# First attention chunk's low halves moved from GpSimd to VectorE, semaphores, a bank and a tile count moved at the two expert layers

## The chip, the cores and the metric

The kernel runs on one core of a Trainium2 chip. The metric is device time in microseconds, lower is better. The four engines that compute (TensorE, VectorE, ScalarE, GpSimd) and SyncE, which issues most transfers, each work through an own queue in program order and meet at semaphores: an instruction waits until a semaphore has reached a value, and raises one when it ends. Chunk, block and tile are used below as the kernel's own units.

## The reference

Three stages, each on 9984 rows of 256 values:

```python
# B=4, S=2496, D=256, z of width 64
attn = maximum(z @ z.T / S, 0) ** 2          # for each of the 4 batches
x    = u * (attn @ v)

# first expert layer: 8 experts, hidden width 1024
do   = x @ w_skip > 0                         # rows that are computed; others pass unchanged
e    = argmax(x @ w_gate);  g = softmax(...)[e]
x    = x + g * (relu(x @ w1[e]) @ w2[e])      # only where do

# second expert layer: the gate has a bias by the row's modality (0 or 1)
e    = argmax(x @ w_gate2 + bias[modality]);  g = softmax(...)[e]
out  = g * (relu(x @ w1b[e]) @ w2b[e])
```

## The kernel before, in words

**Precision.** All large products are made from float32 operands that are split in two parts: a high part, which is a rounding copy (`VH`, `ZH`, `AH`), and a low part, which is the operand minus the high part (`VL`, `ZL`, `AL`). A product is three matmuls: high by high, high by low, low by high. So each operand needs a copy on some engine and a subtraction on some engine.

**Attention.** There are 20 chunks, 5 for each batch; a chunk is 512 columns of the output (448 for a batch's last). The other side is taken in 20 blocks of 128, two at a time, so that a chunk has 10 pairs `p`. For a pair TensorE makes the scores (`scores`, line 1567, six matmuls into `pS`), ScalarE applies ReLU (`relus`, line 742) and square (`squares`, line 751) to each block, VectorE splits each block in `AH` (line 1183) and `AL` (line 1185, in `split`), and TensorE sums `V` times `A` (`sums`, `half_sums`, line 1578; twelve matmuls a block). TensorE runs three pairs ahead with its scores (`AHEAD`). Scores of a pair wait for the ReLUs of the pair before. ScalarE's square of a block waits until VectorE has split the block four before it.

**Where V comes from.** `V` of a batch lies in 20 blocks, cast and subtracted two at a time (index `n`, 0 to 9). SyncE loads batch 0 in five pieces: blocks 0 and 1, blocks 2 and 3 (semaphores `v_first_loaded`), blocks 4 to 9 (`v_loaded`), blocks 10 to 15 (`v_mid_loaded`, issued once `vl_ready` has reached 3, because the raw buffer is reused), and 16 to 19 (issued at `vl_ready` 5). In chunk 0 VectorE makes the high parts: `v_high(0)` before chunk 0's loop, the others after the splits of a pair, as the table `V_AT` says (line 1188). GpSimd makes all ten low parts (`v_low`, line 579), each as soon as its high part is there. TensorE's sums of pair `p` wait for `vl_ready` p + 1. For batches 1 to 3 ScalarE makes the high parts and VectorE the low parts, in both versions. The five parts of `Z` are cast by ScalarE (`z_high`) and subtracted by VectorE (`z_low`) in both.

**First expert layer.** Rows that go to one expert lie together in `token_rows`, and are taken in tiles of 256. The first tile ("lead") is made by `lead_layer1` and `lead_layer2`, written out by hand among the last routing steps; hidden units come in four banks. `lead_layer2(n, bank)` waits for the `n`-th raise of `h_split`. How many tiles each expert has is counted on VectorE (`finish_groups(0)`), which raises `cum_ready`; every engine then reads the counts with `value_load` (line 323 in `end_of`) and loops. On TensorE the order is `lead_layer2(2, 1)`, wait for `cum_ready`, read the first count, `lead_layer2(3, 3)`, loop (layer 1 at line 1834, layer 2 at line 1851).

**Second expert layer.** Tiles of 512, in `second_phase` of each engine. TensorE makes tile 0 with `layer1` (line 1886) into the banks `hring_lead` = pT, pS1, pS0 by turns, and `layer2` (lines 1894 and 1896). Eight blocks `f` of hidden units; `layer1(t, ..., f)` waits for `q.h_split`, which VectorE raises by `NF` = 8 at the head of its own `second_phase` (line 1465), and by one with each `h_low`. Before the second `layer1`, TensorE waits for the last output of the first layer (`PH[0].y_out`; it frees pS1), and behind it come three small matmuls (`prefix_x2`, line 1805) that wait for the one-hot of the last first-layer tile, which VectorE makes in `pick_expert` (lines 1383 to 1392) after it has read a count (line 1492). `place_tile`, `finish_groups(1)` and the low halves follow on VectorE. Counts of the second layer go to SyncE, which pads the end of an expert's rows and then loads tile 1 (`load_x`, line 429). TensorE turns the rows of tile 1 with `transpose_half` (line 1877), half by half, into pT, ScalarE (`take_half`) and VectorE (`low_half`) split them. Before the first half it waits for `h_split` NF + 7, with which VectorE has read pT's last block.

Of the kernel before, what the change touches and what calls it, by code (L numbers as in the profile page):

```python
# [5 lines left out]
F32 = mybir.dt.float32  # L6
# [4 lines left out]
ALU = mybir.AluOpType  # L11
# [5 lines left out]
B, S, D, DQ = 4, 2496, 256, 64  # L17
# [6 lines left out]
KP = KT // 2  # L24
# [5 lines left out]
VU = KT // 2  # L30
# [4 lines left out]
FIRST = 4  # L35
# [3 lines left out]
VHALF = KT // 2  # L39
VMID = VHALF + 6  # L40
# [7 lines left out]
NF = F // P  # L48
# [19 lines left out]
def bass_attention_two_moe(nc, u, v, z, w_skip, w_gate, w1, w2, modality, w_gate2, bias2, w2t, out):  # L68
    xs = nc.dram_tensor("token_rows", (GR * CAP + SPARE, ROW), F32, kind="Internal").ap()

    with ExitStack() as ctx:
# [430 lines left out]
        def _(pool):  # L502
            g_ = nc.gpsimd

            def wait(semaphore, value):

                pool.wait_ge(semaphore, value)
                pool.sem_inc(pool_passed, 1)
# [66 lines left out]

            def v_low(n):
                to, at = 2 * n * D, 2 * (n % (VU // 2)) * D
                wait(vh_ready, n + 1)
                g_.tensor_tensor(VL[:, to:to + 2 * D], vraw[:, at:at + 2 * D], VH[:, to:to + 2 * D].bitcast(F32), ALU.subtract).then_inc(vl_ready, 1)

            def row_meta(idx):
# [14 lines left out]
            pool.sem_inc(x_ready, 2)  # L596
            for n in range(VU):
                v_low(n)
            for g in range(CHUNKS):
# [71 lines left out]
        def _(act):  # L671
# [87 lines left out]
            for g in range(CHUNKS):  # L759
                b, c = divmod(g, QC)  # L760
                n = TAIL if c == QC - 1 else QW
                for p in range(KP):
# [8 lines left out]
                    if g == 0 and p in (1, 2, 4):  # L771
                        z_high(0, 2 + p // 2)
                    if p in MIDDLE and b < B - 1:
                        m = MIDDLE.index(p)
# [130 lines left out]
            def second_phase():  # L905
# [35 lines left out]
                for f in range(NF):  # L941
                    h_high(0, f, hring_lead)
                    if 3 <= f < 3 + WP:
                        split_high(E + 1, 1, f - 3)
                take_half(1, 0, 0, pT[:, :])
                take_half(1, 0, 1, pT[:, :])
                keep_marks(1, 0)
# [47 lines left out]
        def _(dve):  # L995
# [171 lines left out]
            def v_high(n):  # L1167
                w, at = slice(2 * n * D, 2 * (n + 1) * D), 2 * (n % (VU // 2)) * D
                if 2 * n < FIRST:
                    dve.wait_ge(v_first_loaded[n], 16)  # L1170
                elif VHALF <= 2 * n < VMID:
                    dve.wait_ge(v_mid_loaded, 16)
                else:
                    dve.wait_ge(v_loaded, 16 if 2 * n < VHALF else 64)
                v_.tensor_copy(VH[:, w], vraw[:, at:at + 2 * D]).then_inc(vh_ready, 1)
# [11 lines left out]

            V_AT = {0: (1,), 1: (2, 3), 2: (4,), 4: (5,), 5: (6, 7), 6: (8,), 7: (9,)}
            final_done = [0]
# [53 lines left out]

            z_low(0, 0)
            v_high(0)
            z_low(0, 1)
            for g in range(CHUNKS):
                n = TAIL if g % QC == QC - 1 else QW
                for p in range(KP):
                    split(g, p, n)  # L1250
                    if g == 0:
                        if p in (1, 2, 4):
                            z_low(0, 2 + p // 2)
                        for m in V_AT.get(p, ()):
                            v_high(m)
                    else:
# [47 lines left out]
            dve.sem_inc(PH[0].h_split, 4)  # L1304
            dve.sem_inc(PH[0].y_out, 1)
            dve.wait_ge(u_loaded, 16 * CHUNKS)
# [155 lines left out]
            def second_phase():  # L1462

                q = PH[1]
                dve.sem_inc(q.h_split, NF)
                dve.sem_inc(q.y_out, 1)

# [33 lines left out]
                for f in range(3, NF):  # L1501
                    h_low(0, f, hring_lead)
                low_half(1, 0, 0, pT[:, :])
                low_half(1, 0, 1, pT[:, :])
                dve.wait_ge(marks_loaded, 16)
# [38 lines left out]
        def _(pe):  # L1544
# [246 lines left out]
            for ph in range(1):  # L1791
# [4 lines left out]
                gate_columns(1)  # L1796
                lead_layer2(2, 1)
                pe.wait_ge(cum_ready, ph + 1)
                first_end = end_of(pe, 0, 0)
                lead_layer2(3, 3)  # L1800

# [65 lines left out]
            def second_phase():  # L1867
# [66 lines left out]
                layer2(0, 0, 4)  # L1934
                pe.wait_ge(q.h_split, NF + 7)
                transpose_half(1, 0, pT)
                layer2_last(0, 0, lambda: transpose_half(1, 1, pT))
                pe.wait_ge(cum_ready, 2)
# [62 lines left out]
```

## Time and profile before

| what | us |
|---|---|
| timed runs, median of 3 | 1475.42 (1475.3 to 1476.66) |
| profiled execution | 1478.75 |
| its span | 1477.20 |
| TensorE busy | 1454.6 (98%) |
| VectorE busy | 980.9 (66%) |
| ScalarE busy | 778.2 (53%) |
| GpSimd busy | 278.9 (19%) |
| granted TensorE clock, share of full speed | 0.998 |

The span is the time from the first to the last instruction of the profiled execution; 1.55 us lie around it. The profiled execution is 3.3 us over the median of the timed ones. In the rows PE is TensorE's matmuls and PEld its weight loads, DVE is VectorE, ACT ScalarE, POOL GpSimd, SP SyncE; a name with q behind it is an engine's queue of register, branch and semaphore instructions. A bracket [0.28 <-ACT R L742] says that the engine stood idle for 0.28 us before the row and what ended that. "issue" is a wait that no semaphore in the profile explains. The ends of matmuls are modelled.

### The profile page before, as it was taken

The numbers are of one execution on the slowest core, as the hardware profiler recorded it, in microseconds if no ns is written. First come the engines' busy times: TensorE is split into PE (matmuls) and PEld (weight loads), VectorE is DVE, ScalarE is ACT, GpSimd is POOL, SyncE is SP. The second block draws the span as 40 slices with busy tenths as digits, with TensorE's granted clock in tenths as the row PEclk, the third lists the DMA queues.
The fourth block names the chain that finished last, engine by engine and source line by source line (L and its number), as shares of the span: only waits on it lengthen the run. The fifth ranks groups of instructions, "written<-read, shape, count | busy, mean of one in ns | idle before, by whom it ended". The sixth has DMA issues, their size and how long they took to land.

```text
span 1477.2 us, 34369 instructions
## 1 busy us (share of the span) xinstructions
PE 1454.6 (98%) x11832; PEld 1312.6 (89%) x11832; DVE 980.9 (66%) x2487; ACT 778.2 (53%) x1540; POOL 278.9 (19%) x309
## 2 busy tenths in 40 slices
PE   9999999999999999999999999999999999999997
PEld 7889998999998898889899999997888888888885
DVE  7988888888788888888676666674333333333332
ACT  6677767677667677666444444444333333333332
POOL 4011111111111111111332222225121121211212
PEclk9999999999999999999999999999999999999999
DMA  5311030201311111031464344323111121111110
GB/s 122 101 52 45 30 101 29 66 31 43 101 63 39 38 50 67 31 102 58 131 211 131 129 142 133 107 97 124 47 43 47 40 73 43 43 47 40 58 44 26
DMA packets 59066, 108.01 MB, mean 73 GB/s; under 512 B 18615, under 2 KB 33474, under 8 KB 58940
## 3 DMA queue, kind: packets, MB, share of 16 engines
q1 hardware_dynamic: 40396, 47.46, 11.5%
q0 software_dynamic: 18544, 58.96, 11.4%
q8 instruction: 69, 1.13, 0.3%
q14 instruction: 57, 0.47, 0.1%
HBM read 75.61 MB, written 32.31 MB: 73 GB/s over the span
## 4 chain that ended last, share of the span: by engine, by line
PE 95%; issue 2%; DVE 1%; ACT 0%; DMA 0%; SPq 0%; POOLq 0%; DVEq 0%; POOL 0%; ACTq 0%
PE pO L1578 33%; PE pS L1886 11%; PE pO L1894 10%; PE pS L1567 9%; PE pS L1851 9%; PE pO L1834 9%; PE pO L1896 5%; PE pM L1886 4%; PE pT L1877 1%; PE pO L1587 1%; PE pM L1650 1%; DVE AH L1183 1%; PE pT L1769 1%; PE pO L1751 0%; PE pS L1738 0%
## 5 line engine op out<-in xcount | busy, mean ns | idle before, releaser
L1578 PE MATMUL pO<-AH,VH 64*128 64x512 f32 (+1 forms) x1520 | 323.8, 383 | 0.8 <-DVE AL L1185 0.5
L1578 PE MATMUL pO<-AH,VL 64*128 64x512 f32 (+1 forms) x1520 | 322.9, 382 | 1.7 <-issue 1.7
L1578 PE MATMUL pO<-AL,VH 64*128 64x512 f32 (+1 forms) x1520 | 323.1, 382 | 0.0
L742 ACT ACTIVATE R<-pS 128x512 f32<-128x512 f32 (+1 forms) x400 | 213.7, 589 | 168.3 <-PE pS L1567 165.6
L1185 DVE TENSOR_TENSOR AL<-A,AH 128x512 fp32r<-128x512 f32 (+1 forms) x400 | 278.9, 697 | 13.7
L751 ACT ACTIVATE A<-R 128x512 f32<-128x512 f32 (+1 forms) x400 | 228.2, 626 | 9.0 <-DVE AL L1185 9.0
L1894 PE MATMUL pO<-VL,AH 128*128 128x512 f32 x640 | 232.2, 400 | 0.0
L1183 DVE CAST AH<-A 128x512 fp32r<-128x512 f32 (+1 forms) x400 | 170.5, 426 | 45.7 <-ACT A L751 45.2
L1578 PEld LDWEIGHTS pO<-AH,VH 64*128 64x128 f32 x1520 | 172.2, 184 | 15.8 <-issue 1.5
L1578 PEld LDWEIGHTS pO<-AH,VL 64*128 64x128 f32 x1520 | 172.4, 184 | 15.2 <-issue 2.9
L1578 PEld LDWEIGHTS pO<-AL,VH 64*128 64x128 f32 x1520 | 172.4, 184 | 12.5
L1477 DVE SCALAR_TENSOR_TENSOR AL<-pS,AH 128x512 fp32r<-128x512 f32 x119 | 82.2, 691 | 150.9 <-ACT AH L924 150.9
L1896 PE MATMUL pO<-VL,AL 128*128 128x256 f32 x640 | 179.1, 280 | 0.0
L1886 PE MATMUL pS<-ZH,VH 128*128 (+1 forms) x476 | 160.6, 391 | 0.0
L924 ACT ACTIVATE AH<-pS 128x512 fp32r<-128x512 f32 x119 | 71.2, 599 | 163.4 <-PE pS L1886 134.0
L631 POOL DMA_INDIRECT out_dram<-xrow,tok_at x80 | 78.1, 977 | 366.7 <-DVE xrow L1487 354.3
L1894 PEld LDWEIGHTS pO<-VL,AH 128*128 128x128 f32 x640 | 120.2, 188 | 26.4
L1896 PEld LDWEIGHTS pO<-VL,AL 128*128 128x128 f32 x640 | 120.4, 188 | 2.4
L1834 PE MATMUL pO<-ZH,VH 128*128 x704 | 117.3, 284 | 0.1
L1851 PE MATMUL pS<-VL,AH 128*128 128x264 f32 x704 | 116.0, 287 | 0.0
L1886 PEld LDWEIGHTS pS<-ZH,VH 128*128 128x128 f32 x476 | 89.4, 188 | 20.3
L1834 PEld LDWEIGHTS pO<-ZH,VH 128*128 128x128 f32 x704 | 98.5, 191 | 1.4 <-issue 1.4
(276 smaller groups left out, 2387.4 us busy)
## 6 DMA issues: line engine op xcount, KB each, us to landing
raw<-in_w_dram POOLq DMA_DIRECT2D x22, 1024.0 KB
A<-token_rows SPq DMA_DIRECT2D x20, 536.0 KB
uT<-in_u_dram SPq DMA_DIRECT2D x16, 512.0 KB, 3.7
xin<-token_rows SPq DMA_DIRECT2D x23, 268.0 KB
raw<-in_v_dram SPq DMA_DIRECT2D x8, 768.0 KB
A<-in_w2t_dram POOLq DMA_DIRECT2D x8, 512.0 KB
raw<-in_z_dram SPq DMA_DIRECT2D x8, 368.0 KB, 5.0
token_rows<-pad_row SPq DMA_DIRECT2D x8, 268.0 KB
```

Of the source, the lines that this page charges most:

```text
L742: s_.activation(R[k % 2][:, 0:n], pS[k % 2][:, 0:n], ACT.Relu, scale=1.0 / S).then_inc(relu_done, 1)
L751: s_.activation(A[k % NA][:, 0:n], R[k % 2][:, 0:n], ACT.Square).then_inc(square_done, 1)
L1183: v_.tensor_copy(AH[k % NBUF][:, 0:n], A[k % NA][:, 0:n]).then_inc(ah_ready, 1)
L1185: v_.tensor_tensor(AL[k % NBUF][:, 0:n], A[k % NA][:, 0:n], AH[k % NBUF][:, 0:n].bitcast(F32), ALU.subtract).then_inc(al_ready, 1)
L1477: v_.scalar_tensor_tensor(out=AL[f][:, :], in0=ring[f % RING][:, :], scalar=0.0, in1=AH[f][:, :].bitcast(F32), op0=ALU.max, op1=ALU.subtra ...
L1567: last = t_.matmul(pS[r][:, 0:n], w[rows, (2 * p + r) * P:(2 * p + r + 1) * P], x[rows, zc:zc + n], start=(m == 0), stop=(m == 2))
L1578: last = t_.matmul(pO[:, (KD * r + d) * QW:(KD * r + d) * QW + n], vv[rows, vo + k * D + d * P:vo + k * D + (d + 1) * P], a[k % NBUF][rows ...
L1834: last = t_.matmul(pO[:, bank * 512 + fi * TT:bank * 512 + (fi + 1) * TT], w[h][:, kd, f * P:(f + 1) * P], x[:, ds(par, 1), kd, :].rearran ...
L1851: last = t_.matmul(pS[s][:, 0:width], a[p][:, fi * TT + s * P:fi * TT + (s + 1) * P], w[h][:, f, 0:width], start=(f == 0 and n == 0), stop ...
L1886: last = t_.matmul(ring[f % RING][:, :], w[h][:, kd, f * P:(f + 1) * P], x[:, ds(par, 1), kd, :].rearrange("p o t -> p (o t)"), start=(n = ...
L1894: t_.matmul(pO[:, s * QW:(s + 1) * QW].rearrange("p (m d) -> p m d", m=2), AH[f][:, rows], w2hl[h][:, :, f, 0:D], start=(f == 0), stop=(f ...
L1896: return t_.matmul(pO[:, s * QW:s * QW + D], AL[f][:, rows], w2h[h][:, f, 0:D], start=False, stop=(f == NF - 1), skip_group_check=True)
```

## The change

1. Attention, chunk 0: GpSimd's ten `v_low` are gone. VectorE makes them in its own order, `v_low(0, 0)` before its loop and `v_low(0, p + 1)` after the splits of pair p. VectorE keeps `v_high(0)` and `v_high(1)`; the high parts 2 to 9 are made by ScalarE, `v_high(0, p + 1)` after the squares of pair p, for p = 1 to 8.
2. VectorE raises `PH[1].h_split` by 8 and `PH[1].y_out` by 1 before the first expert layer, no longer at the head of `second_phase`.
3. Tile 1 of the second layer is turned into pM instead of pT. TensorE's wait before it is for `PH[0].base` of the last first-layer tile (pM's last reader) instead of `h_split` NF + 7.
4. TensorE makes `lead_layer2(3, 3)` before it waits for `cum_ready` and reads the first count.

```diff
...
@@ GpSimd @@
-            def v_low(n):
-                to, at = 2 * n * D, 2 * (n % (VU // 2)) * D
-                wait(vh_ready, n + 1)
-                g_.tensor_tensor(VL[:, to:to + 2 * D], vraw[:, at:at + 2 * D], VH[:, to:to + 2 * D].bitcast(F32), ALU.subtract).then_inc(vl_ready, 1)
...
-            for n in range(VU):
-                v_low(n)
@@ ScalarE, chunk loop @@
                     if g == 0 and p in (1, 2, 4):
                         z_high(0, 2 + p // 2)
+                    if g == 0 and 1 <= p < KP - 1:
+                        if p == 1:
+                            act.wait_ge(vh_ready, 2)
+                        v_high(0, p + 1)
@@ ScalarE, second layer @@
-                take_half(1, 0, 0, pT[:, :])
-                take_half(1, 0, 1, pT[:, :])
+                take_half(1, 0, 0, pM[:, :])
+                take_half(1, 0, 1, pM[:, :])
@@ VectorE @@
             def v_high(n):
...
-                if 2 * n < FIRST:
-                    dve.wait_ge(v_first_loaded[n], 16)
-                elif VHALF <= 2 * n < VMID:
-                    dve.wait_ge(v_mid_loaded, 16)
-                else:
-                    dve.wait_ge(v_loaded, 16 if 2 * n < VHALF else 64)
+                dve.wait_ge(v_first_loaded[n], 16)
...
-            V_AT = {0: (1,), 1: (2, 3), 2: (4,), 4: (5,), 5: (6, 7), 6: (8,), 7: (9,)}
...
             z_low(0, 0)
             v_high(0)
+            v_low(0, 0)
             z_low(0, 1)
...
-                        for m in V_AT.get(p, ()):
-                            v_high(m)
+                        if p == 0:
+                            v_high(1)
+                        if p < KP - 1:
+                            v_low(0, p + 1)
...
             dve.sem_inc(PH[0].h_split, 4)
-            dve.sem_inc(PH[0].y_out, 1)
+            dve.sem_inc(PH[1].h_split, NF)
+            for q in PH:
+                dve.sem_inc(q.y_out, 1)
...
                 q = PH[1]
-                dve.sem_inc(q.h_split, NF)
-                dve.sem_inc(q.y_out, 1)
...
-                low_half(1, 0, 0, pT[:, :])
-                low_half(1, 0, 1, pT[:, :])
+                low_half(1, 0, 0, pM[:, :])
+                low_half(1, 0, 1, pM[:, :])
@@ TensorE @@
                 lead_layer2(2, 1)
+                lead_layer2(3, 3)
                 pe.wait_ge(cum_ready, ph + 1)
                 first_end = end_of(pe, 0, 0)
-                lead_layer2(3, 3)
...
-                pe.wait_ge(q.h_split, NF + 7)
-                transpose_half(1, 0, pT)
-                layer2_last(0, 0, lambda: transpose_half(1, 1, pT))
+                pe.wait_ge(PH[0].base, total0 + 1)
+                pe.sem_inc(pe_passed, 1)
+                transpose_half(1, 0, pM)
+                layer2_last(0, 0, lambda: transpose_half(1, 1, pM))
```

## Rows read from the trace of the kernel before

**Rows 1.** The page's part 4: shares of the chain that ended last, by engine
```profile
PE 95%; issue 2%; DVE 1%; ACT 0%; DMA 0%; SPq 0%; POOLq 0%; DVEq 0%; POOL 0%; ACTq 0%
```

**Rows 2.** The chain in order of time: start us, us, engine, group
```profile
49.87 3.06 PE pO L1578 x24
...
56.33 0.68 PE pS L1567 x6
...
732.90 4.38 PE pS L1851 x36
```

**Rows 3.** Timeline of TensorE, chunk 0: start us, us, engine, line, operation, count [idle before]
```profile
11.08 0.51 PE L1578 MATMUL pO<-AH,VH 64*128 64x512 f32 x2
...
14.65 0.46 PE L1567 MATMUL pS<-ZH 64*128 64x512 f32 x2
...
17.24 0.50 PE L1567 MATMUL pS<-ZH 64*128 64x512 f32 x2 [0.28 <-ACT R L742]
...
19.41 0.45 PE L1567 MATMUL pS<-ZH 64*128 64x512 f32 x2
```

**Rows 4.** Timeline of VectorE, chunk 0
```profile
15.86 0.76 DVE L1175 CAST VH<-raw 128x512 fp32r<-128x512 f32 x2
...
20.12 0.69 DVE L1185 TENSOR_TENSOR AL<-A,AH 128x512 fp32r<-128x512 f32 x1
```

**Rows 5.** Groups by line and shape, first 60 us: busy us, mean ns, idle
```profile
L1185 DVE TENSOR_TENSOR AL<-A,AH 128x512 fp32r<-128x512 f32 x30 | 27.6, 919 | 1.0
...
L579 POOL TENSOR_TENSOR VL<-raw,VH 128x512 fp32r<-128x512 f32 x10 | 13.3, 1337 | 20.8 <-DVE VH L1175 20.8
```

**Rows 6.** TensorE at the count of the first layer: its queue's load, then its timeline
```profile
L323 PEldq TENSOR_LOAD <-cum x1: 572/572/572, 720.8 to 720.8; - x1
...
721.80 0.33 PE L1738 MATMUL pS<-VL,AH 128*128 128x264 f32 x1
...
724.99 0.39 PE L1834 MATMUL pO<-ZH,VH 128*128 x2
```

**Rows 7.** Timelines of TensorE and VectorE, start of the second layer
```profile
1002.79 0.50 PE L1886 MATMUL pT<-ZH,VH 128*128 128x512 f32 x1 [1.34 <-DVEq L1465]
...
1003.73 0.17 DVE L1383 TENSOR_SCALAR take<-xrow 128x2 f32<-128x2 f32 x1 [0.74 <-DVE xrow L1456]
...
1005.25 0.17 DVE L1392 TENSOR_TENSOR oh<-eq,take 128x16 bf16<-128x16 f32 x1
```

**Rows 8.** Timeline of TensorE and waits of SyncE's queue, before tile 1
```profile
1022.54 0.63 PE L1877 MATMUL pT<-ident,A 128*128 128x128 f32 x4 [1.23 <-issue]
...
SPq L439 <- DVE pad_from L1342: 13.6, 1, 13.6
```

**Rows 9.** Windows: from:to us, length, busy PE, PEld, DVE, ACT, POOL, PEclk, DMA, GB/s
```profile
8.00:9.00 1.00, 0.57 (x10) 0.40 (x8) 0.74 (x1) 1.00 (x3) 0.34 (x1) 1.00 0.93 220
...
13.90:14.00 0.10, 0.10 (x6) 0.06 (x4) 0.10 (x1) 0.10 (x2) 0.00 (x0) 1.00 0.11 31
...
1021.90:1022.00 0.10, 0.00 (x0) 0.00 (x0) 0.00 (x0) 0.00 (x0) 0.10 (x1) 1.00 0.22 86
```

**Rows 10.** Timeline of ScalarE, chunk 0
```profile
14.45 1.15 ACT L751 ACTIVATE A<-R 128x512 f32<-128x512 f32 x2
...
15.49 0.62 ACT L721 CAST ZH<-raw 128x512 fp32r<-128x512 f32 x1
...
16.00 1.10 ACT L742 ACTIVATE R<-pS 128x512 f32<-128x512 f32 x2
...
16.97 1.17 ACT L751 ACTIVATE A<-R 128x512 f32<-128x512 f32 x2
```

**Rows 11.** VectorE's queue at the start of the second layer, lines 1465 and 1492
```profile
L1465 DVEq EVENT_SEMAPHORE  x1: 21/21/21, 1002.7 to 1002.7; - x1
...
L1492 DVEq TENSOR_LOAD <-cum x1: 310/310/310, 1002.9 to 1002.9; - x1
```

**Rows 12.** TensorE's queue, line 323, the second layer's count
```profile
L323 PEldq TENSOR_LOAD <-cum x1: 336/336/336, 1025.5 to 1025.5; - x1
```

## The prediction

> **What bounds the kernel now.** I read the page first, then the chain in order of time, then the timelines of single engines where TensorE stands. The chain that ended last is TensorE for 95% [rows 1]. So only time in which TensorE stands still, or in which its matmuls come further apart than they must, can be won. There are three such places that the change touches.
>
> Place one is the first attention chunk. The chain in order of time runs through VectorE there, and TensorE takes it over only at 49.87 us, with the first sums of chunk 1; from then on a set of six matmuls (scores of two blocks, or half of one block's sums) takes 0.68 us without a break [rows 2]. TensorE's first sums start at 11.08 [rows 3]. Between the two lie 50 such sets: 8 of scores before chunk 1's, 3 of chunk 1's, and 39 of sums (16 blocks of 2, and 7 single ones for the last four blocks). 50 x 0.683 = 34.1 us; they take 38.8, so 4.7 us are lost. Why, a timeline row and a group say: a subtraction on VectorE takes 0.69 us by itself [rows 4], but 0.919 on average over the first 60 us, in which GpSimd makes its ten subtractions of 1.34 us each [rows 5]. 30 x 0.23 = 6.9 us of VectorE's time go there.
>
> Place two is the end of the first expert layer's first tile, at 721 to 725 us: TensorE's sequencer reads the tile count for 0.57 us, and the twelve matmuls behind it take from 721.80 to 724.99, where line 1834 starts [rows 6]. Matmuls of that kind take 0.12 us (4.38 for 36) [rows 2], so 1.46; 1.7 us are lost.
>
> Place three is the start of the second layer: 1.34 us of idle before 1002.79, released by VectorE's semaphore at line 1465 [rows 7], and 1.23 us before the turning of tile 1 at 1022.54 [rows 8].
>
> **Part 1, chunk 0: 0.7 us won.** GpSimd's ten subtractions go. VectorE gets them: 10 x 0.69 = 6.9 us; it gives up 8 casts (two take 0.76, so 3.0) [rows 4] and the 6.9 us of stretching. A pair of blocks then costs it 2 x (0.4 + 0.69) for the splits and 0.69 for the subtraction, 2.9 us, under TensorE's 5 x 0.683 = 3.4. VectorE stops being the bound.
>
> But ScalarE now makes the eight casts, and its queue is in order: the cast of V's third piece stands ahead of the ReLUs of blocks 4 and 5, and must wait for that piece's load. The load is not waited for in the old trace. Its last bytes move at 13.9 to 14.0 us [rows 9]; later, tile 1's load ends at 1022.0 and TensorE, which waited for it, starts at 1022.54 [rows 8, 9], so half a microsecond passes from bytes to semaphore. I take 14.5. The bounds are 14.0 (no delay) and 15.86, where VectorE casts the same piece without having waited [rows 4].
>
> From there, with ScalarE's steps of 0.97 for two ReLUs, 1.04 for two squares, 0.51 for a cast [rows 10], and 0.15 from a ReLU's end to the scores:
> cast at 14.5, ReLUs 4 and 5 from 15.0 to 16.1, next scores at 16.25 (before: 14.65);
> squares 15.97, casts 17.0 and 17.5, ReLUs 18.0 to 19.1, next scores at 19.27 (before: 17.24);
> squares 19.0, cast 20.0, ReLUs 20.5 to 21.6, next scores at 21.8 (before: 19.41) [rows 3].
> TensorE idles for about 1.5, 0.9 and 0.4 us, where it idled 0.28 once. After that ScalarE needs 2.0 + 0.5 + at most 0.5 us in each 3.4 and runs ahead; V's later pieces are asked for no later than now, since the subtraction that frees the raw buffer ends by about 16.3 in these steps, and GpSimd's could not start before the cast at 15.86 and took 1.34. So from 21.8 there are 40 sets left: 21.8 + 0.08 + 40 x 0.683 = 49.2, against 49.87. Won: 0.7, and by the bounds 1.2 or a loss of 0.7. Nothing later absorbs it: up to the end of the first layer TensorE is the chain.
>
> The gaps in that stretch leave TensorE busy for 4.1 of 7 us. A row nearby: from 8 to 9 us it was busy 0.57 of the time and the granted clock was 1.00 [rows 9]. I therefore charge nothing for the clock. The Trainium skill (TensorE: Matmul & The Clock Gate, section HAM oscillation) says that idle gaps between bursts of matmuls can put the array back to the lower of its two rates. By that rule this part would lose; the trace does not agree so far, and the rival below has its price.
>
> **Part 2, the second layer's start: 0.2 us won.** The idle 1.34 us goes, but not the time. The first of the freed steps starts at about 1001.5 and needs 1.5 us; the next waits for the last tile's output, which VectorE ends at 1002.99 (the 0.74 us before the row at 1003.73 count from there), so it starts at 1003.15 and ends at 1004.6. Then comes the prefix matmul, which waits for the one-hot that VectorE ends at 1005.42 [rows 7]. In the old trace it ran at 1005.66 (1002.79 + 1.50 + 6 x 0.228), with nothing to wait for. So the wait moves to the one-hot. What is really won is VectorE's: its two semaphore instructions (0.1 us each, from 1002.7 to the count's load at 1002.9) no longer stand before that load [rows 11], so the one-hot, the counts and all that hangs on them come 0.2 us sooner. Bounds: 0 and 0.4.
>
> **Part 3, the other bank for tile 1: 0.** The stall ends with tile 1's rows, not with a free bank. SyncE waits for VectorE's counts [rows 8], pads, and loads; the last bytes come at 1022.0 [rows 9]. Bank and wait change nothing of that. TensorE's new wait (the first layer's last base) is long met by then, and pM's next writer, the third matmul block of tile 1, already waits for both splits. The 0.2 us above pass through, and no more: had TensorE come earlier it would have stood longer here.
>
> **Part 4, the count read later: 0.5 us won.** The nearest row for "load behind the matmuls, loop next" is the second layer's own count, at 1025.5: 0.34 us, fully hidden by queued matmuls [rows 12]. That speaks for all of the 1.7 us. Against it: the sequencer's load, its twelve pairs of instructions and the loop's entry are one queue whose sum stays the same; only if the stutter comes from the load itself is it saved, and the load is 0.57 of it. An empty queue at the loop's entry could cost that 0.57, with the register work behind it 0.9. I take 0.5, between 1.7 won and 0.9 lost, near the 0.57 of the load's own row [rows 6]. What is late next, the second tile's load, is not near.
>
> **Sum.** 0.7 + 0.2 + 0 + 0.5 = 1.4 us. The profiled execution took 1478.75 us (span 1477.20 and 1.55 around it), so it would take 1477.35. The timed runs, whose median is 1475.42, are 3.3 us below it; the difference carried over gives 1474.0. About 0.2% (3 us) is what a measurement of this kernel can tell from no change.
>
> **Rivals.**
> A, the cover is thinner: the load lands at the upper bound, or ScalarE's chain takes a little more per step, and part 4 costs 0.2. Then +0.7 - 0.2 + 0.2 = +0.7: 1476.1. For it: chunk 0's first 10 us have no slack on ScalarE. Chance 0.18.
> B, all of it comes: the load is early (1.2), part 2 gives 0.3, the stutter was the load's (1.7): 3.2 us, 1472.2. For it: the row at 1025.5. Against it: three independent ends of three ranges. Chance 0.15.
> C, slower: the clock falls in chunk 0 between 14.5 and 22 us. About 5.5 us of matmuls there would take twice as long, +5.5 - 1.4 = +4.1: 1479.5. It decides from the point at which the row of the granted clock goes below 1. Against it: 1.00 in every slice, also at 0.57 busy. Chance 0.06.
> D, the change doesn't do what it says at the second layer's start, since the one-hot takes over the wait: this is my forecast, and the rival that the 1.34 us are won whole (a further 1.1, so 1472.9) has 0.04; the rest is the forecast, 0.57.
>
> **The numbers.** 1474.0 is the likeliest case. Its own range is about 1472.8 to 1475.4. For 8 in 10 I take in A and most of B: 1471.9 to 1476.8. Faster by over 0.2% (under 1472.5) needs nearly all of B: 0.14. Slower needs C or something unseen: 0.06. Within: 0.80.
>
> **What would show it.** In chunk 0 ScalarE idle before its first cast of V (line 733) until about 14.5; TensorE gaps near 16, 19 and 22 and none from there to 60; VectorE's subtractions all at 0.69; chunk 1's first sums near 49.2. At the second layer: no idle before its first matmul, a short one at the second step and about 0.7 before the prefix, which stays near the one-hot's end; the stall before tile 1's turning still over 1 us. At the first layer: line 1834 starting up to 1.7 us sooner after the last block (B) or not (A). Wrong would be a granted clock under 1, a TensorE gap in chunk 0 after 25 us, or a second layer that starts over 0.5 us sooner against VectorE's last tile.

## The result and the profile after

The changed kernel takes 1478.24 us (median of 17 runs, 1476.70 to 1480.58) against 1475.30 (17 runs, 1474.45 to 1476.66): 1.0020 times as long, 95% interval 1.0013 to 1.0026. The forecast was 1474.0 with a range up to 1476.8. Its profiled execution took 1478.14 us with a span of 1476.3, like its other runs. That of the kernel before took 3.45 us more than this median: between the first sums of chunk 1 and the last of attention its TensorE needs 656.3 us, 2.6 more than the changed kernel's 653.7, in code that the change leaves alone. So the two spans (1477.2 and 1476.3) don't show the loss. The places do.

The page of the changed kernel, parts 1, 2 and 4:

```profile
span 1476.3 us, 34361 instructions
...
PE 1453.8 (98%) x11832; PEld 1297.1 (88%) x11832; DVE 978.0 (66%) x2489; ACT 781.6 (53%) x1548; POOL 266.6 (18%) x299
...
PEclk9999999999999999999999999999999999999998
...
PE 96%; DMA 1%; issue 1%; DVE 1%; SPq 1%; ACT 0%; POOLq 0%; DVEq 0%; POOL 0%; ACTq 0%
```

The chain is TensorE's, as in [rows 1]. The clock row is too coarse to show what follows.

**Chunk 0** came as forecast. TensorE's scores and its first sums of chunk 1 in the timeline of the changed kernel, to be held against [rows 2, 3]:

```profile
16.10 0.50 PE L1561 MATMUL pS<-ZH 64*128 64x512 f32 x2 [1.34 <-ACT R L735]
...
19.25 0.50 PE L1561 MATMUL pS<-ZH 64*128 64x512 f32 x2 [0.79 <-ACT R L735]
...
21.69 0.50 PE L1561 MATMUL pS<-ZH 64*128 64x512 f32 x2
...
49.14 0.39 PE L1572 MATMUL pO<-AH,VH 64*128 64x512 f32 x2
```

The prediction's steps had 16.25, 19.27, 21.8 and 49.2. ScalarE waits for V's third piece until 14.45 (forecast 14.5), here in its timeline:

```profile
14.45 0.62 ACT L726 CAST VH<-raw 128x512 fp32r<-128x512 f32 x1 [1.20 <-DMA raw<-in_v_dram]
```

And VectorE's subtractions are as short as forecast, here as groups by line and shape over the first 60 us (against 0.919 us in [rows 5]):

```profile
L1177 DVE TENSOR_TENSOR AL<-A,AH 128x512 fp32r<-128x512 f32 x30 | 20.8, 692 | 1.0
L1128 DVE TENSOR_TENSOR VL<-raw,VH 128x512 fp32r<-128x512 f32 x10 | 6.9, 686 | 0.1
```

**The first layer's count** did not. TensorE's timeline of the changed kernel there, against [rows 6]:

```profile
720.29 0.37 PE L1732 MATMUL pS<-VL,AL 128*128 128x264 f32 x1 [0.45 <-issue]
...
722.10 0.50 PE L1828 MATMUL pO<-ZH,VH 128*128 x2 [0.72 <-issue]
```

The stutter (single matmuls with gaps between them that no semaphore explains, at 721.8 to 724 us in [rows 6]) is still there, now ahead of the read, and a further 0.72 us of idle stands before the loop. From the last of attention's sums to the loop's first matmul it takes 19.3 us, against 18.8 before.

**The second layer.** Timeline of TensorE, the last group of the first layer and then what the change touches, against [rows 7, 8]:

```profile
998.13 0.40 PE L1845 MATMUL pS<-VL,AL 128*128 128x264 f32 x2
998.37 0.39 PE L1880 MATMUL pT<-ZH,VH 128*128 128x512 f32 x1
...
1000.20 0.47 PE L1880 MATMUL pS<-ZH,VH 128*128 128x512 f32 x1 [0.28 <-DVE xrow L1452]
...
1002.37 0.18 PE L1799 MATMUL pM<-oh,before 128*128 128x16 bf16 x1 [0.54 <-DVE oh L1388]
...
1020.08 0.75 PE L1871 MATMUL pM<-ident,A 128*128 128x128 f32 x4 [2.09 <-DMA A<-token_rows]
```

Counted from the last group, the prefix matmul comes at 4.24 us (before: 1005.66 less 1001.06 = 4.60), so TensorE wins 0.36 us. But tile 1's rows come later: at 21.95 us, against 21.48. The stall grows from 1.23 to 2.09 us. And then this, in the windows of the changed kernel (columns as in [rows 9], the granted clock third from the end):

```profile
1019.00:1020.00 1.00, 0.00 (x0) 0.00 (x0) 0.00 (x0) 0.00 (x0) 0.48 (x1) 1.00 0.36 146
1020.00:1021.00 1.00, 0.92 (x5) 0.89 (x6) 0.00 (x0) 0.13 (x1) 0.75 (x1) 0.75 0.00 0
1021.00:1022.00 1.00, 1.00 (x5) 0.85 (x4) 0.52 (x1) 0.45 (x1) 0.98 (x2) 0.50 0.50 33
1022.00:1023.00 1.00, 1.00 (x5) 0.81 (x5) 0.18 (x1) 0.00 (x0) 0.00 (x0) 0.50 0.51 147
1023.00:1024.00 1.00, 1.00 (x5) 0.90 (x4) 0.00 (x0) 0.00 (x0) 0.00 (x0) 0.54 1.02 422
```

After the stall, at about 1020.5, the granted clock falls to 0.50, 1.2 GHz, for some 3 us. From tile 1's turning to the last matmul it takes 445.00 us, against 443.44 before: 1.56 us more, which I put down to the clock. In the kernel before the same windows show 1.00 throughout.

Why the rows come later stands in the timelines of VectorE and GpSimd, changed kernel:

```profile
1008.62 2.56 POOL L550 TENSOR_TENSOR VH<-raw,VH 128x512 fp32r<-128x512 f32 x2 [0.70 <-ACT VH L707]
...
1008.70 1.24 DVE L1335 TENSOR_SCALAR cum<-sums 128x9 int32<-128x9 f32 x1
```

VectorE writes the counts, nine numbers, in 1.24 us. In the kernel before the same two rows stand the other way round:

```profile
1011.81 0.17 DVE L1339 TENSOR_SCALAR cum<-sums 128x9 int32<-128x9 f32 x1
...
1011.96 2.56 POOL L550 TENSOR_TENSOR VH<-raw,VH 128x512 fp32r<-128x512 f32 x2 [0.92 <-ACT VH L714]
```

Freed by the semaphores, VectorE comes 0.2 us sooner to this write and GpSimd 0.4 us sooner to its subtraction (through ScalarE's cast, for which it waits), so the order of the two is reversed (times from the last group of the first layer, at 1001.06 and 998.13: the write at 10.75 and 10.57, the subtraction at 10.90 and 10.49). The write ends at 1009.94, when the first of GpSimd's two subtractions (1.28 us each) is over.

### The profile page after: what moved, and what is told of

Same layout as the page of the kernel before. It is cut to its first block, busy times and chain, and to the rows that moved or that the text cites. A ratio compares the mean times of both kernels' runs of the same rounds, so it can differ in the third digit from the quotient of the medians.

```text
span 1476.3 us, 34361 instructions
## 1 busy us (share of the span) xinstructions
PE 1453.8 (98%) x11832; PEld 1297.1 (88%) x11832; DVE 978.0 (66%) x2489; ACT 781.6 (53%) x1548; POOL 266.6 (18%) x299
## 4 chain that ended last, share of the span: by engine, by line
PE 96%; DMA 1%; issue 1%; DVE 1%; SPq 1%; ACT 0%; POOLq 0%; DVEq 0%; POOL 0%; ACTq 0%
PE pO L1572 34%; PE pS L1880 11%; PE pO L1888 10%; PE pS L1561 9%; PE pS L1845 9%; PE pO L1828 9%; PE pO L1890 5%; PE pM L1880 4%; PE pT L1871 1%; PE pO L1581 1%; PE pM L1644 1%; PE pT L1763 1%; DMA raw<-in_v_dram 0%; PE pO L1745 0%; PE pS L1732 0%
## 5 line engine op out<-in xcount | busy, mean ns | idle before, releaser
L1572 PE MATMUL pO<-AH,VL 64*128 64x512 f32 (+1 forms) x1520 | 314.2, 382 | 1.8 <-issue 1.8
L1572 PE MATMUL pO<-AL,VH 64*128 64x512 f32 (+1 forms) x1520 | 314.3, 382 | 0.0
L1572 PE MATMUL pO<-AH,VH 64*128 64x512 f32 (+1 forms) x1520 | 314.2, 382 | 0.0
L1177 DVE TENSOR_TENSOR AL<-A,AH 128x512 fp32r<-128x512 f32 (+1 forms) x400 | 272.2, 680 | 13.7
L1572 PEld LDWEIGHTS pO<-AH,VL 64*128 64x128 f32 x1520 | 163.2, 184 | 19.5 <-issue 2.9
L1572 PEld LDWEIGHTS pO<-AH,VH 64*128 64x128 f32 x1520 | 163.3, 184 | 17.7 <-issue 0.5
L1572 PEld LDWEIGHTS pO<-AL,VH 64*128 64x128 f32 x1520 | 163.5, 184 | 17.2
```

The lines of the kernel that those rows point to most:

```text
L1177: v_.tensor_tensor(AL[k % NBUF][:, 0:n], A[k % NA][:, 0:n], AH[k % NBUF][:, 0:n].bitcast(F32), ALU.subtract).then_inc(al_ready, 1)
L1572: last = t_.matmul(pO[:, (KD * r + d) * QW:(KD * r + d) * QW + n], vv[rows, vo + k * D + d * P:vo + k * D + (d + 1) * P], a[k % NBUF][rows ...
```

## The experiments

Theory S: the loss is made by part 2: counts late through GpSimd, a longer stall at tile 1, a fallen clock. Theory O: it is made elsewhere, by part 1 or part 4. Four more letters stand in the expectations: K (idling is what makes the clock fall), H (stops and stutter go with the chip), and, for what the changed kernel loses on the slower chips beyond that, L (part 1 costs there what it gives) and M (part 4 makes it). Two kinds of chips came up. On two of them the kernel before takes 1470.4 us, on two others 1475.5, as in the comparison above. All times of a run are set against the kernel before on the same chip. The changed kernel itself was timed on the slower kind alone.

A low mean clock of a run is a hint and no proof of a fallen clock at one of the places: in every profile the clock is at 0.50 for the last 6 to 9 us of the span too, after the last matmul, and three runs of part 1 alone have a mean of 0.996 at 1470.24, 1470.38 and 1470.78 us, beside others of 1469.74 to 1470.49.

**Part 1 alone**

```diff
-            for n in range(VU):
-                v_low(n)
...
+                    if g == 0 and 1 <= p < KP - 1:
+                        if p == 1:
+                            act.wait_ge(vh_ready, 2)
+                        v_high(0, p + 1)
...
+                        if p < KP - 1:
+                            v_low(0, p + 1)
```

> Part 1 alone (chunk 0 without GpSimd's subtractions). Theory S (the loss of the change comes at the second layer's tile 1, where a stall of 2.1 us makes the clock fall): chunk 1's first sums at 49.1 to 49.2 us, granted clock 1.00 up to the end of the matmuls, stall before tile 1's turning 1.2 us as before, time 0.7 us below the kernel before. Theory O (the loss comes from the gaps in chunk 0, through the clock or through stops elsewhere in attention): 1 us or more above it.

Measured: 1470.12 against 1470.47 us, ratio 0.9999 (0.9990 to 1.0008); of the 0.7 us expected 0.35 show. The medians of the spans differ by 0.5 us (1468.4 and 1468.9); 0.2 us more than before lies around the span (1.79 and 1.59). Clock 1.00 and a stall of 1.07 us before tile 1. It was run a second time, on a chip of the 1475 us kind:

> Part 1 alone again. On a chip of the 1470 us kind: 0.4 us below the kernel before, as on the first such chip. On one of the 1475 us kind, theory L (part 1 costs there what it gives, since V's third piece comes later or the stops are more): 0.5 to 1.5 us above the kernel before; theory M (the unexplained 2 us of the changed kernel there come from part 4): 0.4 us below it.

1475.18 against 1475.45 us, 0.9998 (0.9989 to 1.0007). V's third piece came later here, at 15.06, and TensorE idled 1.86 us; its timeline and one window:

```profile
16.71 0.50 PE L1561 MATMUL pS<-ZH 64*128 64x512 f32 x2 [1.86 <-ACT R L735]
```

```profile
15.00:16.00 1.00, 0.00 (x0) 0.00 (x0) 1.00 (x3) 0.94 (x2) 0.00 (x0) 1.00 0.00 0
```

Even so the clock stayed at 1.00. Part 1 shows no loss on either kind: theory L falls, and so does O for this part.

**Part 2 alone**

```diff
             dve.sem_inc(PH[0].h_split, 4)
-            dve.sem_inc(PH[0].y_out, 1)
+            dve.sem_inc(PH[1].h_split, NF)
+            for q in PH:
+                dve.sem_inc(q.y_out, 1)
...
-                dve.sem_inc(q.h_split, NF)
-                dve.sem_inc(q.y_out, 1)
```

> Part 2 alone (second layer's semaphores raised early). Theory S: no idle before the second layer's first matmul, the stall before tile 1's turning grows from 1.2 to about 1.6 us if tile 1's rows come as long after the last first-layer matmul as before, and to 2.1 us if VectorE's write of the counts is drawn out by GpSimd's casts (1.24 us in the changed kernel, 0.17 before); in the second case the clock falls for some 3 us and the time is 1.5 to 3 us above the kernel before. Theory O: within 0.4 us of the kernel before, mostly below it.

Measured: 1471.99 against 1470.47 us, 1.0011 (1.0002 to 1.0020), on a chip of the faster kind. The write of the counts takes 1.23 us, with GpSimd's subtraction 0.08 ahead of it; tile 1 is turned 22.05 us after the last group (21.30 in the run of part 4 alone on this chip), behind a stall of 2.21. In the profiled run the clock did not fall. The 11 runs lie from 1471.11 to 1471.99 (six) and from 1472.23 to 1472.94 (five); the three with a mean clock of 0.996 are among the five. So S holds for the counts: even the fastest of these runs is 0.6 us above the median before. That the clock adds to it in some is what their times and mean clocks suggest; no profile shows one of the longer runs.

**All but part 2**: the two semaphores raised at the head of the second phase again, the rest of the change kept.

> The changed kernel with the two semaphores back at the head of the second phase (parts 1, 3 and 4 stay). Theory S: TensorE idles 1.3 us before the second layer, stall before tile 1 1.2 us, clock 1.00 there, time about 0.2 us below the kernel before (0.7 won in chunk 0, 0.5 lost at the count), so 3 us below the changed kernel. Theory O: as slow as the changed kernel, 3 us above the kernel before.

Measured: 1470.08 against 1470.47 us, 0.9997 (0.9988 to 1.0006). The stall is 0.78 us (expected 1.2), the write 0.17. Without part 2 there is no loss on this chip; on the slower kind this kernel was not run.

**Part 4 alone**

```diff
-                pe.wait_ge(cum_ready, ph + 1)
-                first_end = end_of(pe, 0, 0)
                 lead_layer2(3, 3)
+                pe.wait_ge(cum_ready, ph + 1)
+                first_end = end_of(pe, 0, 0)
```

> Part 4 alone (the first count read behind the last hand-written block). Theory S: the dribble of the matmuls stays where it is and a further 0.7 us of idle stands before the loop's first matmul, 0.5 us above the kernel before. Theory O, with the loss here: 2 us or more above.

1470.48 against 1470.47 us, 1.0001 (0.9992 to 1.0010); the expected loss of 0.5 is not there. There is no stutter on this chip, with the count early or late: from attention's last sums to the loop it takes 16.80 us both ways. On a chip of the slower kind:

> Part 4 alone again. On a chip of the 1470 us kind: no difference. On one of the 1475 us kind: theory M 1.5 to 2.5 us above the kernel before, theory L 0.5 us above it, which is what the profile of the changed kernel shows at the count.

1476.38 against 1475.45 us, 1.0006 (0.9997 to 1.0015): 0.9 us, between L and M, and by its interval not clear of nothing; three of eleven runs took 1477.6 or more. The profiled one (1477.63) is one of these, and its windows and TensorE's timeline say why:

```profile
719.00:720.00 1.00, 0.75 (x4) 0.42 (x4) 0.00 (x0) 0.00 (x0) 0.59 (x1) 1.00 0.20 73
720.00:721.00 1.00, 0.60 (x5) 0.52 (x5) 0.00 (x0) 0.37 (x1) 0.00 (x0) 1.00 0.82 277
721.00:722.00 1.00, 0.48 (x4) 0.27 (x3) 0.29 (x1) 0.00 (x0) 0.00 (x0) 0.93 0.21 67
722.00:723.00 1.00, 0.57 (x2) 0.57 (x3) 0.92 (x5) 0.00 (x0) 0.00 (x0) 0.50 0.00 0
723.00:724.00 1.00, 1.00 (x7) 1.00 (x6) 0.00 (x0) 0.00 (x0) 0.00 (x0) 0.50 0.00 0
```

```profile
722.43 0.79 PE L1834 MATMUL pO<-ZH,VH 128*128 x2 [0.95 <-issue]
```

The read takes 0.73 us and starts 1.9 us ahead of the loop's first matmul; in the run of part 4 alone without the stutter it takes 0.49 and starts 2.2 ahead, and no idle shows. As I read it, the stutter empties TensorE's queue just ahead of the read, so the read, which is covered where there is no stutter, adds 0.95 us of idle. The clock fell within that gap, at about 721.9. The stutter and the gap do not always bring this: in the changed kernel's profile TensorE is busy for 0.52, 0.71 and 0.38 of the microseconds from 719 to 722, no more than here, and the clock stays at 1.00. Of the six profiles with the late read on the slower kind it fell here in two. The kernel before on the same chip, a run of its own:

> The kernel before itself once more, for a profile beside the next three. On a chip of the kind on which it takes 1475 us it shows the unexplained short stops of TensorE in attention and the dribble at the first count; on one of the kind with 1470 us neither. Theory H expects on the first kind some 691 to 693 us from chunk 0's first sums to the end of attention, as the changed kernel has there.

It has the stutter too (gaps of 0.23, 0.32 and 0.34 us), but the queue is full again at the loop:

```profile
720.91 0.37 PE L1738 MATMUL pS<-VL,AL 128*128 128x264 f32 x1 [0.34 <-issue]
...
721.85 0.41 PE L1834 MATMUL pO<-ZH,VH 128*128 x2
```

From attention's last sums to the loop it takes 18.35 us here and 19.55 with the late read. Over all profiles of the slower kind it is 18.35 to 18.82 with the early read (four) and 19.28 to 19.55 with the late one (six), so the order costs time there. From chunk 0's first sums to the loop it takes 710.92 us on this chip, and 705.55 on one of the faster kind, which is the run for which theory H had been written down:

> The kernel before itself, for a profile on the same chip as the next three. Theory H (the short stops in attention that no semaphore explains, and the dribble at the first count, come and go with the chip and not with the change): on a chip where the next three show them this one does too, and from chunk 0's first sums to the end of attention it takes within 1 us of theirs plus the 0.7 us of chunk 0. Rival (the change itself brings them in attention): it takes 3 us less than that.

It showed no stops and no stutter, and nor did the variants on that chip. On the slower kind the kernel before has them where the changed one has (the stops near 168, 201, 341 and 514 us). So H holds: they go with the chip, and not with the change. These stretches hold the 5 us between the two kinds.

**The changed kernel again, and three cures**, on one chip of the slower kind, each cure an edit of the changed kernel. GpSimd held, with one wait ahead of its subtractions:

```diff
             scatter_rows(total)
+            wait(cum_ready, 2)
             next_weights(E, 0, True)
```

Filler, ahead of the wait for tile 1's rows:

```diff
+                for _i in range(8):
+                    t_.matmul(pM[:, :], w1h[0][:, 0, 0:P], XTH2[:, 1, 0, :], start=True, stop=True)
                 transpose_half(1, 0, pM)
```

Turning later, where the third argument of the second call replaces its wait for the first half's split (it has a bank of its own; ScalarE and VectorE read pT for it):

```diff
-                transpose_half(1, 0, pM)
-                layer2_last(0, 0, lambda: transpose_half(1, 1, pM))
+                layer2_last(0, 0, lambda: (transpose_half(1, 0, pM), transpose_half(1, 1, pT, 2)))
```

> The changed kernel itself, beside the kernel before and the next three. By the four runs before (part 1 -0.35 us, part 2 +1.5, part 4 0.0, parts 1, 3 and 4 together -0.4) the sum is 1.1 to 1.2 us above the kernel before; the earlier pair of the two kernels had 2.9. If the difference is the clock (theory K: a stall of over 2 us leaves it at the edge), single runs scatter upwards by 1 us and more and show a lower mean clock where they are longer; if it is something fixed, they don't.

> The changed kernel with GpSimd's low halves of the second expert's weights held until VectorE has written the counts (one wait). Theory S (the counts are late because GpSimd's subtraction starts 0.1 us before VectorE's row of line 1335): that row takes 0.17 us instead of 1.24, the pad and load of tile 1 are issued 1.0 us sooner after the last first-layer matmul, its turning comes at 20.6 instead of 21.8 us after it, the stall before it falls from 2.1 to 1.0 us, no run shows a fallen clock there, and the time is 1.1 us (what came late) and up to 1.4 more (the clock) below the changed kernel. Rival: the row is long for another reason; then nothing changes.

> The changed kernel with eight matmuls more (128 by 512, 0.23 us each, 1.8 us) just ahead of TensorE's wait for tile 1's rows; they write a bank that is then overwritten. Theory K (idle of 2 us, then a fallen clock): the rows come as late as in the changed kernel, 21.8 us after the last first-layer matmul, but idle is only 0.3 us, the clock stays at 1.00 in every run, and the time is that of the changed kernel's fastest runs, with less scatter. Rival (the clock falls for another reason than idling): no difference in time or scatter.

> The changed kernel with both halves of tile 1 turned behind the second of the four row groups of layer2_last, the second half into pT (24 matmuls of 4.2 us in all; 2.1 us of them now run ahead of the turning). Theory S: the rows, 2.1 us late for TensorE, are then just there: no stall over 0.3 us at the turning, and one of at most 0.6 us at tile 1's first matmul, which waits for the splits; 1.5 to 2 us below the changed kernel, more where its clock falls. Rival: the splits end too late behind the remaining 2.1 us of matmuls, and the stall only moves to tile 1's first matmul (1.5 us or more there).

| run | median us | range | ratio to before (1475.56), interval | stall before tile 1 | turned after last group |
|---|---|---|---|---|---|
| changed again | 1479.36 | 1478.21 to 1481.44 | 1.0024 (1.0015 to 1.0033) | 2.55 | 22.41 |
| GpSimd held | 1477.12 | 1475.41 to 1478.90 | 1.0010 (1.0001 to 1.0019) | 1.37 | 21.22 |
| filler | 1477.71 | 1476.85 to 1478.93 | 1.0013 (1.0004 to 1.0022) | under 0.2 | 21.80 |
| turned later | 1475.76 | 1475.07 to 1477.39 | 1.0000 (0.9991 to 1.0009) | 0.19 | (moved) |

With GpSimd held, VectorE's and GpSimd's timelines read:

```profile
1008.59 0.17 DVE L1336 TENSOR_SCALAR cum<-sums 128x9 int32<-128x9 f32 x1
...
1009.12 2.55 POOL L550 TENSOR_TENSOR VH<-raw,VH 128x512 fp32r<-128x512 f32 x2 [1.30 <-DVE pad_from L1339]
```

The write is short again and the rows come 1.19 us sooner than in the changed kernel beside it (expected 1.2): that GpSimd's subtraction draws the write out is shown. The filler leaves the write at 1.25 us and covers the idle time alone; its timeline, and one window of it and of the changed kernel on the same chip:

```profile
1019.15 2.00 PE L1932 MATMUL pM<-ZH,VH 128*128 128x512 f32 x8
1021.27 0.66 PE L1871 MATMUL pM<-ident,A 128*128 128x128 f32 x4
```

```profile
1022.00:1023.00 1.00, 1.00 (x7) 0.92 (x6) 0.42 (x1) 0.55 (x1) 1.00 (x2) 1.00 0.00 0
```

```profile
1024.00:1025.00 1.00, 1.00 (x5) 0.81 (x5) 0.00 (x0) 0.00 (x0) 0.00 (x0) 0.50 0.98 406
```

Eight useless matmuls make the kernel 1.65 us faster. The rows came 0.6 us sooner in that profile, half of it from an earlier load issue; the larger part is what the clock costs: from the turning to the end it is 443.44 us again, against 445.01. That all eleven of the changed kernel's runs have a mean clock of 0.995 or 0.996, and only four of the filler's, fits. K holds for tile 1. But runs with a mean clock of 0.996 and less remain with all three cures, which the filler's expectation had ruled out. All three still have part 4, and the profile of the kernel that turns later (1477.39 us, its slowest run) shows the other place, behind the loop's start at 722.67:

```profile
724.00:725.00 1.00, 1.00 (x7) 1.00 (x6) 0.00 (x0) 0.00 (x0) 0.00 (x0) 0.50 0.00 0
```

Turning later won 3.6 us on the changed kernel, where 1.5 to 2 and more for the clock were expected.

**Part 4 undone, and the best version**, on a chip of the faster kind.

> The changed kernel with part 4 undone (the first count read ahead of the last hand-written block). Theory S: on a chip whose profile shows the dribble there, attention's end to the loop takes 18.8 us instead of 19.3 and the time is 0.5 us below the changed kernel's; on one without it, 16.8 either way and no difference. The stall before tile 1 of 2.1 us or more stays, so the kernel stays 1 to 3 us above the kernel before. Rival: the order costs nothing anywhere (19.3 stays).

1470.79 against 1470.39 us, 1.0006 (0.9997 to 1.0015), stall 2.26. It was expected to stay 1 to 3 us above the kernel before, and the median is only 0.4 above. Seven runs of 1470.49 to 1470.97 have a mean clock of 0.997 or 0.998; four of 1471.82 to 1472.44 all have 0.996. The means of the two groups lie 1.5 us apart, which is the price of the clock in the profiles; the profiled run is one of the seven, so that the clock fell in the four is inferred.

The next one joins parts 1 and 2, the bank pM, GpSimd held and the later turning, with the count read early:

> Parts 1 and 2 and the bank pM of part 3, with both cures: GpSimd held until the counts are written, both halves of tile 1 turned behind two row groups; the first count read early again. Theory S: no fallen clock in any run, tile 1's turning met without a stall, its rows (20.6 us after the last first-layer matmul) even before TensorE asks. Against the kernel before: 0.5 us won in chunk 0, 0.4 at the start of the layer, 1.2 at tile 1: 2.0 us below it. Rival: what the cures give is lost behind (splits of tile 1 too late, weights too late as GpSimd starts 0.5 us later): within 0.5 us of the kernel before.

1469.11 us, 0.9990 (0.9981 to 0.9999), no run above 1469.54. 1.3 us are won rather than 2.0: tile 1's turning meets no stall, but tile 2's now waits 0.84 us for its load. That load is issued 1.6 us sooner after the last group than with part 1 alone (23.96 and 25.56 us), and TensorE comes 1.5 us sooner to it; in between, from 1017 to 1024 us, the DMA engines are busy throughout (share 0.94 to 1.05) in both. The last one also gives the cast that waited back to VectorE:

```diff
-                    if g == 0 and 1 <= p < KP - 1:
-                        if p == 1:
-                            act.wait_ge(vh_ready, 2)
+                    if g == 0 and 2 <= p < KP - 1:
+                        if p == 2:
+                            act.wait_ge(vh_ready, 3)
...
-                        if p == 0:
-                            v_high(1)
+                        if p in (0, 1):
+                            v_high(p + 1)
...
-                dve.wait_ge(v_first_loaded[n], 16)
+                dve.wait_ge(*((v_first_loaded[n], 16) if 2 * n < FIRST else (v_loaded, 16)))
```

> As the run before, and V's third high part (blocks 4 and 5) cast by VectorE instead of ScalarE, so that no ReLU stands behind the load of that piece. Theory S: ScalarE no longer idles 1.2 us ahead of its first cast of V, TensorE's gaps of 1.3 and 0.8 us near 16 and 19 us shrink to under 0.5 each, and the time is 1.0 to 1.5 us below the run before. Rival (VectorE has no room for the cast there): the gaps move to VectorE's splits, and at most 0.3 us is won.

1467.70 against 1470.39 us, 0.9984 (0.9975 to 0.9993). Its timelines of ScalarE and then of TensorE:

```profile
15.15 0.62 ACT L715 CAST ZH<-raw 128x512 fp32r<-128x512 f32 x1
15.75 0.62 ACT L727 CAST VH<-raw 128x512 fp32r<-128x512 f32 x1
```

```profile
17.50 0.50 PE L1562 MATMUL pS<-ZH 64*128 64x512 f32 x2 [0.87 <-ACT R L736]
...
1011.69 0.60 PE L1872 MATMUL pM<-ident,A 128*128 128x128 f32 x4
1012.13 0.60 PE L1872 MATMUL pT<-ident,A 128*128 128x128 f32 x4
...
1022.18 0.65 PE L1872 MATMUL pT<-ident,A 128*128 128x128 f32 x4 [0.47 <-DMA A<-token_rows]
```

One gap of 0.87 us is left of two, more than the forecast 0.5, and 1.4 us are won as forecast. Two of its eleven runs still took 1469.57 and 1470.38, with a mean clock of 0.996; where it fell in them no profile shows. On a chip of the slower kind:

> The best version again, on another chip. On one of the 1470 us kind 2.7 us below the kernel before. On one of the 1475 us kind by theory M 2.5 us below, since it reads the count early; by theory L 1 us below, since V's third piece no longer holds the ReLUs but the rest of part 1 is in it.

1473.11 against 1475.45 us, 0.9982 (0.9973 to 0.9991). It beats the kernel before on both kinds of chips, by 2.3 and 2.7 us; all its runs here have a mean clock of 0.997 or more. On the faster kind the changed kernel was not timed.

## Why the prediction was wrong, step by step

- **Chunk 0 (0.7 won): the mechanism and its times were right.** Chunk 1's first sums came at 49.14 for a forecast 49.2. In the timed runs only 0.35 and 0.27 us show, inside the noise; 0.2 us of the difference is lost outside the span (1.79 us around it for 1.59), and no run shows why. Rival C (the clock falls here) did not happen, not even at 1.86 us of idle.
- **The second layer's start (0.2 won): right as far as it went, wrong in where it stopped.** The one-hot did take over the wait, and TensorE's prefix came 0.36 us sooner. The step that failed is the sentence that "all that hangs on them come 0.2 us sooner". I moved VectorE and ScalarE and did not look at what GpSimd does beside them. The counts' write stood 0.15 us ahead of GpSimd's subtraction, and an advance of 0.2 on one side and 0.4 on the other put it behind. Price: 1.07 us on the write, 0.9 at the pad's issue, 0.5 to 0.9 at tile 1's rows, where the forecast had a gain of 0.2. The trace of before held both starts, at 1011.81 and 1011.96.
- **The other bank (0):** with it the loss or gain is nil, 1470.08 and 1470.12 us with parts 1, 3 and 4 and with part 1 alone (in their profiles the rows are turned 21.02 and 21.31 us after the last group, which the times do not tell apart). Right. But its sentence "the stall ends with tile 1's rows" missed the stall's own price: behind stalls of up to 1.37 us the clock stayed up in every profile, behind 2.09 it fell in this one, for 1.56 us. The failed term is the clock at tile 1, put at nothing. I had seen that TensorE would wait longer there if it came earlier, and had charged the clock only in chunk 0.
- **The count read later (0.5 won): the wrong sign.** The stutter does not come from the read; it stays when the read moves. On chips that have it the late read costs 0.5 us (first pair of profiles) to 1.2 (18.35 and 19.55), where my bound for a loss was 0.9, and the clock besides in some runs. On the others the read is covered either way. What makes the stutter is open. The row at 1025.5 [rows 12], which I had as speaking for a gain, is a place without a stutter ahead of it.
- **The sum** on the slower kind of chip: -0.3 (part 1) + 0.9 (part 4, with its clock) + 0.5 to 0.9 (rows late) + 1.6 (clock) = 2.7 to 3.1 us, for 2.9 and 3.8 measured. The 0.7 left in the second case has no run of its own. The terms come from different chips, and the interval of part 4's includes zero. The same sum is too low for the kernel with GpSimd held, too: -0.3 + 0.9 and rows 0.3 sooner make 0.3 us, and 1.6 were measured; its four fastest runs (1475.41 to 1476.18) fit 0.3, the other seven are longer, as they would be if the clock fell somewhere, but none of those was profiled. On the faster kind, by the times of the kernels with part 2, the clock at tile 1 falls in a part of the runs only, and there is no stutter.
- **Range and chances.** The price of a fallen clock stood in rival C at 5.5 us for one place, at 0.06. The mechanism deserved a look at every idle stretch that the change lengthens. The Trainium skill (TensorE: Matmul & The Clock Gate, section HAM oscillation) describes the like: waits for a load between bursts of matmuls send the array back to its lower rate, and the next tile starts slow. The windows at 1020 to 1024 us agree in the effect, with 0.50; the waits of the section's example are longer than the 2.09 us here, and than any gap of chunk 0, so that the prediction's "by that rule this part would lose" went further than the page.

## What to carry to other kernels

Before advancing one engine, list what the other engines do beside the instructions that move, with their start times: a tiny write on VectorE 0.15 us ahead of a long GpSimd subtraction is a collision that waits to happen. Idle time of TensorE is not priced by its length alone: ask of each stall what it grows to, and where it grows, move matmuls in front of the wait; even useless ones paid here. And measure an edit of 0.1% on more than one chip: reading the count late cost nothing on a chip without the stutter and some 0.9 us, with an interval that includes zero, on one that has it.

## What the runs showed of the hardware that was not expected

- A VectorE write of nine numbers took 1.24 us instead of 0.17 when it started 0.08 us behind a GpSimd subtraction with two operands in SBUF; it ended with that subtraction. The Trainium skill (SBUF — State Buffer, section Who interferes with whom) says that a `tensor_scalar` can run in a mode with two ports, and that in such a mode it is blocked for the whole of a GpSimd instruction that was issued first. The rows agree in the length; which mode it ran in they don't show.
- Chunk 0's subtractions were stretched from 0.69 to 0.92 us on average by the same kind of neighbour.
- The clock fell behind 2.09 and 2.55 us of idle at tile 1, but not behind 2.21 and 2.26 in two profiled runs, and not behind 1.86 in chunk 0. It also fell at the count, where no gap was over 0.95 us and TensorE had been busy for 0.75, 0.60 and 0.48 of three microseconds, but not in the changed kernel's profile, with 0.52, 0.71 and 0.38. So neither the gap nor the busy share tells by itself when it falls; what decides is open.
- One and the same kernel takes 1470.4 us on two chips and 1475.5 on two others. The slower ones have short stops (0.3 to 0.6 us, unexplained by any semaphore) in attention and the stutter at the count. What makes them was not tried.
